# Eleven buffers for the normalised rows of attention, and the MLP's first rows prepared inside the last expert tile

## The reference

```python
# attention: 8 heads of 64; heads 0-3 see the 32 positions before, heads 4-7 every 32nd position
scores = scale * np.matmul(q, k.transpose(0, 1, 3, 2))
scores = np.where(masks[None], scores, -1e9)
scores = scores - np.max(scores, axis=-1, keepdims=True)
attn = np.exp(scores)
attn = attn / (np.sum(attn, axis=-1, keepdims=True) + 1e-09)
x = np.matmul(attn, v)            # rearranged to (2304, 512)
# experts: rows with x @ w_skip > 0 go to one of 8 experts, the others pass through
h = np.maximum(x[mask] @ w1[e], 0.0)
out[mask] = x[mask] + gate_w[mask, None] * (h @ w2[e])
# MLP, 512 -> 2048 -> 512
h = out @ w_in
g = np.maximum(0.01 * h, h)
return g @ w_out
```

## Time and profile before

| | |
|---|---|
| timed runs, median (lowest to highest) | 775.16 us (774.77 to 778.14), 3 runs |
| the profiled execution: its time | 770.74 us |
| its span, first to last instruction | 768.8 us |
| TensorE, matmuls busy | 719.7 us (94%) |
| VectorE, ScalarE, GpSimd busy | 276.0, 231.6, 182.8 us |
| mean granted TensorE clock | 0.973 of full speed |

### The profile page before, as it was taken

One profiled execution on the slowest core, in us unless ns is written; L12 is line 12 of the kernel. 1 busy time (PEld: TensorE's weight loads), 2 busy tenths in 40 slices (PEclk: granted clock), 3 DMA queues, 4 the chain that ended last, 5 costly groups with the idle time before them and its releaser, 6 DMA issues.

```text
span 768.8 us, 12332 instructions
## 1 busy us (share of the span) xinstructions
PE 719.7 (94%) x4674; PEld 670.2 (87%) x4674; DVE 276.0 (36%) x597; ACT 231.6 (30%) x505; POOL 182.8 (24%) x173
## 2 busy tenths in 40 slices
PE   4979999594989999998999999999999999999997
PEld 3969999583989999997999999999999999899986
DVE  5736667467431111113233223323222322232222
ACT  2645676251111111112222322222222232223222
POOL 5231110002267777764000300110030002001000
PEclk9988999796899999999999999999999999999999
DMA  8475755852777999961000200010020002001001
GB/s 177 111 176 123 179 144 156 245 183 67 239 227 259 318 311 319 310 225 58 3 1 1 83 0 1 29 55 1 0 74 8 0 7 75 0 0 42 1 1 41
DMA packets 68648, 81.68 MB, mean 106 GB/s; under 512 B 26137, under 2 KB 47417, under 8 KB 68602
## 3 DMA queue, kind: packets, MB, share of 16 engines
q1 hardware_dynamic: 60040, 58.60, 25.5%
q0 software_dynamic: 7504, 22.44, 9.0%
q10 hardware_dynamic: 1058, 0.02, 0.1%
HBM read 68.84 MB, written 12.21 MB: 105 GB/s over the span
## 4 chain that ended last, share of the span: by engine, by line
PE 83%; DMA 6%; DVE 4%; SPq 2%; issue 2%; ACT 1%; POOL 0%; ACTq 0%; DVEq 0%; POOLq 0%
PE psum L1643 26%; PE psum L1661 26%; PE psum L1537 9%; PE psum L1553 8%; DMA x_rows<-xo 5%; PE psum L1414 3%; PE psum L1435 2%; PE psum L1386 2%; SPq L447 1%; PE psum L1476 1%; PE psum L1493 1%; PE psum L1424 1%; PE psum L1563 1%; PE psum L1625 1%; PE psum L1405 1%
## 5 line engine op out<-in xcount | busy, mean ns | idle before, releaser
L1353 DVE SCALAR_TENSOR_TENSOR g_act<-g_raw 128x384 f32<-128x384 f32 x96 | 53.5, 558 | 230.9 <-ACT g_raw L1004 230.9
L1643 PE MATMUL psum<-x2h,wih 128*128 128x384 f32 x384 | 130.6, 340 | 2.4 <-DVE x2l L1335 2.4
L1643 PE MATMUL psum<-x2h,wil 128*128 128x384 f32 x384 | 129.4, 337 | 0.0
L1643 PE MATMUL psum<-x2l,wih 128*128 128x384 f32 x384 | 128.9, 336 | 0.0
L1004 ACT ACTIVATE g_raw<-psum 128x384 f32<-128x384 f32 x96 | 47.2, 492 | 235.6 <-PE psum L1643 235.6
L1661 PE MATMUL psum<-woh,g_l 128*128 128x512 f32 x288 | 114.0, 396 | 0.0
L1661 PE MATMUL psum<-wol,g_h 128*128 128x512 f32 x288 | 113.8, 395 | 0.0
L1661 PE MATMUL psum<-woh,g_h 128*128 128x512 f32 x288 | 112.2, 389 | 0.6 <-DVE g_l L1357 0.6
L844 POOL DMA_INDIRECT out_dram<-o_sb,idxo x15 | 16.0, 1064 | 294.4 <-ACT o_sb L999 291.3
L1537 PE MATMUL psum<-xt,wring 128*128 128x160 f32 x512 | 82.6, 309 | 0.6 <-issue 0.6
L1553 PE MATMUL psum<-hp,wring 128*128 128x160 f32 x512 | 78.2, 301 | 0.0
(11 more groups left out here) (208 smaller groups left out, 875.8 us busy)
## 6 DMA issues: line engine op xcount, KB each, us to landing
wring<-in_moe_w_dram SPq DMA_DIRECT2D x64, 512.0 KB, 5.7
x_sb<-x_rows SPq DMA_DIRECT2D x4, 1024.0 KB, 7.3
stage<-in_moe_w_in_dram POOLq DMA_DIRECT2D x4, 1024.0 KB, 5.5
stage<-in_moe_w_out_dram POOLq DMA_DIRECT2D x4, 1024.0 KB, 8.2
q_st<-in_q_dram SPq DMA_DIRECT2D x7, 576.0 KB
k_st<-in_k_dram SPq DMA_DIRECT2D x7, 576.0 KB
vs<-in_v_dram SPq DMA_DIRECT2D x20, 128.0 KB, 7.9
x_rows<-xo SPq DMA_DIRECT2D x8, 288.0 KB, 7.0
```

The costliest lines, as they stand in the source:

```text
L1353: dve.scalar_tensor_tensor(out=g_act[:, f % 2, :], in0=g_raw[:, f % 2, :], scalar=LEAK, in1=g_raw[:, f % 2, :], op0=ALU.mult, op1=ALU.max) ...
L1643: last = pe.matmul(bank[f % 2][:, 0:MT * P], wt[:, c, f * P:(f + 1) * P], xp[:, T.par, c, :], start=(c == 0 and n == 0), stop=(c == KD - 1 ...
```

## The change

- `xo` has a slot for each of the 11 groups. `normalised` waits for the store of its own slot of the batch before, no longer for one of its own batch. The regions behind it in SBUF move up by five slots.
- On POOL, in tile 8, the gather of the MLP's first rows comes first, behind a wait for the split before it (s_stl), and ahead of tile 7's put.
- `tile(0, E - 1, ends=True)`: TensorE turns the three row blocks inside it, two behind share 5, one behind share 6, the third into bank 0 instead of bank 7 (`X2T_0`); ScalarE and VectorE split them there, ahead of the copies of y.
- y of tile 8 is turned in the MLP, behind share 0 of its first block (banks 2 and 3); `rows_of_eight` on VectorE is its x2_rows, behind g_l of step 1; POOL's put waits for it (s_r8).
- g_h moves to the second half of `stage`, so ScalarE waits once for the last split; the loads of last_tile and last_par from the plan move into the overflow part, which redoes gather, turn and split (this part, with semaphores s_t2, s_h2, s_l2r, is not entered here and is cut below).

```diff
-    xo = at(a, "xo", [P, NL, 4 * DH])
+    xo = at(a, "xo", [P, NG, 4 * DH])
...
+    m_ = [a2[0] + 2048 * 4]
+    g_h = at(m_, "g_h", [P, 2, MT * P], F32R)
     m_ = [a2[0] + 2 * 2048 * 4]
     o_sb = at(m_, "o_sb", [P, MT, D])
-    g_h = at(m_, "g_h", [P, 2, MT * P], F32R)
+    m_ = [a2[0] + 2 * 2048 * 4 + 2 * 2 * D * 4]
...
+        X2T_0 = [bank[i] for i in (2, 3, 0)]
...
-                src = xo[0:G["m"], g - NL, :]
+                src = xo[0:G["m"], g, :]
...
+                if i == 2 * NU - 1:
+                    pool.wait_ge(s_srt, 16)
+                    pool.wait_ge(s_stl, i)
+                    indices(0)
+                    gather_rows(s_gm)
                 if i == 0:
                     pool.wait_ge(s_xt, 2)
...
-                if i == 2 * NU - 1:
-                    pool.wait_ge(s_srt, 16)
-                    indices(0)
-                    gather_rows(s_gm)
                 stage_split(i)
...
             with pool.Else():
-                pool.sem_inc(s_rd, 1)
-                pool.wait_ge(s_x2r, 2 * E)
+                pool.wait_ge(s_r8, 2)
                 put_x(E - 1)
...
+                if ends:
+                    for j in range(MT):
+                        x2_hi(0, j, 0)
                 act.wait_ge(s_l2, T.n(FC, FC))
...
+                    if T.first and f == 0:
+                        act.wait_ge(s_stl, 2 * NU)
...
-                if o < NL:
-                    dve.wait_ge(s_xs[store_of(o + NL if o + NL < NG else o)], 16 * b + 16)
-                else:
-                    dve.wait_ge(s_xs[store_of(o - NL)], 16 * b + 32)
+                dve.wait_ge(s_xs[store_of(o)], 16 * b + 16)
...
+            def rows_of_eight():
+                dve.wait_ge(s_y8, 2)
+                dve.tensor_copy(gate2[:, :], gate_s[:, 2 * (E - 1):2 * E]).then_inc(s_g8, 1)
+                dve.wait_ge(s_g8, 1)
+                dve.wait_ge(s_yf, E)
+                for hf in range(2):
+                    dve.scalar_tensor_tensor(out=yr[:, hf, :], in0=bank[2 + hf][0:HALF, :],
+                                             scalar=gate2[:, hf:hf + 1],
+                                             in1=xg[:, (E - 1) % 2, hf, :], op0=ALU.mult,
+                                             op1=ALU.add).then_inc(s_r8, 1)
...
+                if ends:
+                    for j in range(MT):
+                        x2_lo(0, j, 0)
                 dve.wait_ge(s_l2, T.n(FC, FC))
...
-            x2_rows(last_tile, last_par, 5)
-            for j in range(MT):
-                x2_lo(0, j, 0)
...
+                    if f == 1 and T.first:
+                        rows_of_eight()
...
+                    if ends and f == FC - 1:
+                        pe.wait_ge(s_x2r, T.n(2, 0))
+                        x2_turn(0, 0)
+                        x2_turn(0, 1)
+                    if ends and f == FC:
+                        x2_turn(0, 2)
...
-            pe.wait_ge(s_yv, last_tile + 1)
-            y_turn(last_tile, 5)
-            pe.wait_ge(s_x2r, last_tile * 2)
-            pe.wait_ge(s_rd, 1)
-            for j in range(MT):
-                x2_turn(0, j)
...
-                    pe.wait_ge(s_x2r, tiles * 2)
...
+                    if T.first and f == 1:
+                        y_turn(E - 1, s_y8)
+                    if T.first and f == 7:
+                        pe.wait_ge(s_r8, 2)
```

More of the change, by code:

```diff
@@ L531, in _, with tile @@
             tiles = sp.value_load(plan[0:1, 31:32], min_val=E, max_val=TILES)
-            def tile(i0, d):
+            def tile(i0, d, ends=False):
                 nxt = i0 + (d + 1)
@@ L551, in _ @@
                     tile(i2 * 2, u + 1)
-            tile(0, E - 1)
+            tile(0, E - 1, ends=True)
             with sp.If(tiles > E):
@@ L967, in _ @@
                     tile(Tile(i2 * 2, u + 1))
-            tile(Tile(0, E - 1), False)
+            tile(Tile(0, E - 1), False, ends=True)
             with act.If(tiles > E):
@@ L1297, in x2_rows, with x2_lo, tile @@
                                              op1=ALU.add).then_inc(s_x2r, 1)
-            def tile(T, ahead=True):
+            def x2_lo(m, j, par, made=s_m3h, done=s_m3l):
+                dve.wait_ge(made, m * MT + j + 1)
+                dve.tensor_tensor(x2l[:, par, :, P * j:P * j + P],
+                                  x2_bank(m, j).rearrange("d (c t) -> d c t", c=KD),
+                                  x2h[:, par, :, P * j:P * j + P].bitcast(F32),
+                                  ALU.subtract).then_inc(done, 1)
+            def rows_of_eight():
[8 more added lines that the diff above has]
+                                             op1=ALU.add).then_inc(s_r8, 1)
+            def tile(T, ahead=True, ends=False):
                 first, par = T.first, T.par
@@ L1562, in y_turn, with x2_turn, tile @@
                     for c in range(KD):
-                        last = pe.transpose(bank[to + hf][0:HALF, c * P:(c + 1) * P],
+                        last = pe.transpose(bank[2 + hf][0:HALF, c * P:(c + 1) * P],
                                             yt[:, c, HALF * hf:HALF * hf + HALF], ident[:, :])
-                    last.then_inc(s_yt, 1)
-            def tile(T, ahead=True):
+                    last.then_inc(s_done, 1)
+            def x2_turn(m, j, landed=None, turned=s_m3):
+                pe.wait_ge((landed or s_gm)[j], m * 16 + 16)
+                for c in range(KD):
+                    last = pe.transpose(x2_bank(m, j)[:, c * P:(c + 1) * P],
+                                        x3[:, j, c * P:(c + 1) * P], ident[:, :])
+                last.then_inc(turned, 1)
+            def tile(T, ahead=True, ends=False):
                 first, par = T.first, T.par
@@ L1599, in _ @@
                     tile(Tile(i2 * 2, u + 1))
-            tile(Tile(0, E - 1), False)
+            tile(Tile(0, E - 1), False, ends=True)
             with pe.If(tiles > E):
+                pe.wait_ge(s_m3l, MT)
                 for hf in range(2):
```

57 lines of the change are left out of this document (32 added, 25 removed).

## The result

| | before | changed kernel |
|---|---|---|
| median, 20 runs each on one chip | 777.27 us | 769.83 us |
| ratio, 95% interval | | 0.9922 (0.9901 to 0.9943) |
| profiled execution: time, span | 770.74, 768.8 us | 769.87, 767.9 us |
| mean granted clock of that execution | 0.973 | 0.973 |

A ratio of 0.9922 is 6.1 us less (4.4 to 7.7); 6.4 us had been forecast, and a time of 768.8. One slow run of the changed kernel (778.85) is left out of the ratio, which stays close to that of the means; the two medians differ by 7.4 us. The two profiled executions differ by 0.9 us only, so the profile has two things to tell: where the gain is, and why this pair hides most of it.

A forecast was written before the change was run, and what follows sets the result against it. Bounds: xo store waits in attention with SP's load queue close behind, and TensorE's waits at the expert-to-MLP seam. Gains 3.8 + 2.6 = 6.4 us, taken off the 775.16 median, gave 768.8 us, own range 767.5 to 769.7.

The forecast's parts named there:

- SP wins 1.3 us: SP's load queue in attention: without two waits for xo, later loads are issued 1.3 us earlier, ends 0 and 1.76.
- Attention without its waits ends near 138 to 140: End of attention: TensorE finishes by 140 and idles from about 138 until batch 0's rows arrive.
- Batch 0's rows at 144.8: Start of routing: batch 0's rows land at 144.8 instead of 146.1, and routing starts there.
- Block 13 at 162.1, 3.8 us won: Routing's first row block needing batch 3 starts at 162.1 instead of 165.95, 3.8 us won out of 16.
- part 1: Attention's end: eleven slots for xo bring 3.8 us, ends 2.6 and 6 us.
- After block 13 routing goes on as before: Rest of routing: stays bound by TensorE as before, so the 3.8 us won at block 13 are kept.
- the clock falls again: Rival at block 13: TensorE's idling brings 1.2 GHz back and takes 5 us, 1.4 us won, 773.8; chance 0.14.
- The signs of being wrong: Last x_load much before 154 or after 156.5, routing's clock low beyond 10 us, or seam over 2 us.
- Gathers and put on POOL cost nothing: POOL in the last tile: earlier gathers hide in idle time, puts hardly move, the split behind starts 4.8 us earlier.
- Turns in the tile 1.34 us, then 1.20 us for the step: Last expert tile: twelve transposes cost 1.34 us; stepping over the not-taken overflow block delays the MLP 1.20 us.
- y in the MLP 0.81 us: MLP behind share 0: eight y transposes cost TensorE 0.81 us in full.
- The seam 2.6 us: Between last expert tile and MLP: 3.43 us earlier start less 0.81 is 2.6 us won, ends 1.4 and 3.2.

The follow-up runs named there:

- run 2: Changed kernel with six xo slots and the old waits for them, so the seam's part alone, against the kernel before: ratio 0.9960, 3.1 us.
- run 1: Kernel before with the eleven xo slots and nothing else, against the kernel before: ratio 0.9955, 3.5 us.
- run 3: Changed kernel without the overflow part (not entered here) and its branch on TensorE; ratio to the kernel before 0.9884.
- run 7: Changed kernel with turns of the identity on TensorE, 30 before block 0 and 12 before block 13; ratio to the kernel before 0.9945.
- run 8: The changed kernel measured once more, nothing altered; ratio to the kernel before 0.9891.
- run 11: Changed kernel with 30 and 12 turns of the identity before blocks 0 and 13, without TensorE's overflow part; ratio to the kernel before 0.9861.
- run 12: run 5 with 20 turns of the identity on TensorE before block 13; ratio to the kernel before 0.9827.
- Run 4: Changed kernel with x_load of batches 0, 1 and 2 issued on ScalarE's queue instead of SP's; ratio to the kernel before 0.9891.
- run 9: run 5 with SP's x_load of batches 0 and 1 moved into batch 2, and of batch 2 to group 4 of batch 3; ratio 0.9859.
- run 10: run 9 without the overflow part on TensorE (not entered here); ratio to the kernel before 0.9876.
- run 5: Changed kernel with the v loads of batch 3's last three groups issued by POOL instead of SP; ratio to the kernel before 0.9860.
- run 6: run 5 without the overflow part on TensorE (not entered here); ratio to the kernel before 0.9866.

## Why the prediction was right, point by point

- *SP wins 1.3 us.* 1.31 in the pair of profiles, by luck: the last x_load was issued at 156.85 and 156.29 with six slots (before, run 2) and at 153.6 to 157.1 with eleven (changed kernel, runs 1, 3, 7, 8 and 11, mean 155.2), so 1.4 us on average with up to 2 to either side from one execution to the next. That the DMA rings are full beside the two gaps of SP's queue, as the prediction has it, no row shows; the rows show issues of 0.8 to 0.9 us there and a DMA share of 0.90 (46 to 53) and 0.95 (80 to 88).
- *Attention without its waits ends near 138 to 140.* Its last values stood at 138.27 to 139.5, but not by TensorE's pace: the v loads of the last groups held it for 4.6 us. The text had SP's queue close behind VectorE for x_load and did not follow it to the v loads. It cost nothing, because x_load was later still.
- *Batch 0's rows at 144.8.* They came at 146.1 in this profile (143.8 in run 8), nothing gained there; it did not matter, as block 13 decides.
- *Block 13 at 162.1, 3.8 us won.* 161.95, 4.0 us; 160.0 to 163.6 over six profiles (those with eleven slots and SP's own order of loads). The step that 12 of 16 us do not arrive was right, and run 1 gives 3.5 us for all of part 1.
- *After block 13 routing goes on as before.* This step failed in three of the four profiles without the turns of the identity and with eleven slots on SP (changed kernel 11.79 us, run 1 10.23, run 3 10.24; run 8 8.66), for 8.57 before. It was the rival "the clock falls again", held at 0.14 and with 5 us; it takes 1.7 us on average of the four. Against that block 13 is 4.3 us early on average of the six, not 3.8, so 2.6 us are left; run 1's interval holds this as well as 3.8. The term of 3.8 us is thus right in size only: the prediction counted the idle time in front of block 13 as free, and it cost clock behind it.
- *The signs of being wrong.* One of them came true in the changed kernel: routing's granted clock is low beyond its first 10 us (routing starts at 146.14, and the clock is 0.53 and 0.50 from 163.5 to 170.4). A second, the last x_load after 156.5, came true in run 1 (157.08). The forecast time held all the same, by luck in so far as the 1.7 us lost behind block 13 are small beside the spread of the timed runs.
- *Gathers and put on POOL cost nothing.* The three gathers went out at 333.65 to 337.4, the split behind the puts began at 340.00 in a tile that stood 1.38 us later than before, so 4.8 us earlier, as forecast.
- *Turns in the tile 1.34 us, then 1.20 us for the step.* From the first of the 24 weight loads to the tile's last it grew from 21.57 to 22.90 us, 1.33; the step took 1.44, and 1.24 to 1.73 over the other profiles that have it. Run 3 shows that it was rightly put on the path: without it the start is 0.9 us earlier.
- *y in the MLP 0.81 us.* 0.87. yr ended at 362.63, the next block's gathers were out by 373.45 (forecast 371.4), and its turns had no wait.
- *The seam 2.6 us.* 3.20 - 0.87 = 2.33 by the trace, 3.1 (1.6 to 4.6) by run 2.
- *Where the profile and the runs differ.* The sum was made against an execution 4.4 us under its median, and only the cut was carried over. That was the right use of it: the first profile pair shows 0.9 us, the pair with run 8 7.9, the timed runs 6.1.

## What to carry to other kernels

When a wait goes, follow the queue that starts the next stage, each kind of transfer on it, before counting the wait as won: here 16 us of idle and slow time at TensorE were 4 us at the block that waits for the last load. Winning in front of such a load buys idle time, and the idle time can cost more than itself in clock; a few cheap matmuls in the gap (run 12) gave back 6.4 us of routing. A timed difference of a few us should be read from many runs and explained from more than one pair of profiles.

## What the runs showed of the hardware

**The clock behind a short idle time.** From block 13 to the last routing row, by the idle time of TensorE in front of block 13: 1.32 us of idle, 8.66 us; 1.45, 11.79; 1.76, 10.24; 2.11, 10.23; 2.23, 11.80; 2.85, 15.09; 3.49, 13.27; 3.90, 13.08. With turns of the identity in the gap (0.64, 1.82 and 0.80 us of idle left) 8.65, 8.66 and 8.66. Run 4 had no idle time there and took 8.60. So each of the seven idle times from 1.45 to 3.90 us without the turns was followed by some 3 to 15 us at 1.2 GHz, and the one of 1.32 was not; 1.32 and 1.45, both of the same kernel, lie so close that what decides between them stays open. Of the changed kernel's timed runs that count in the ratio, those with a mean clock of 0.972 to 0.977 took 765.9 to 771.8 us, those with 0.962 to 0.970 took 773.0 to 777.0; where in those executions the low clock lay, no profile tells.

**Stops of several engines at once.** The four stops of 0.8 to 1.2 us in the expert tiles stood in the first profile of the changed kernel and in runs 9 to 12, and in none of runs 1 to 8, nor in the profile of the kernel before. Run 8 is the changed kernel itself, so its code alone does not make them; runs 1 to 4 and 9 to 11 have the same chip number, 14, so the chip alone does not either. The runs of the kernel before that go with the profiles that have them had medians of 777.27, 776.36 and 776.01, the others 772.09 and 774.12. That the stops cost the kernel before some 4 us there too would fit this and is not shown, as no profile of it has them. POOL does not stop: its issue of the stage load takes 0.83 us (307.50 above), as in run 8 (301.67), and its next instruction follows at once. The cause stays open.

**VectorE's copy beside POOL.** In the second tile a copy of 80x2 numbers takes 4.07 us. VectorE and POOL in the changed kernel:

```profile
215.22 4.52 POOL L658 TENSOR_TENSOR wil<-stage,wih 128x2048 fp32r<-128x2048 f32 x1
215.69 4.07 DVE L1303 COPY gate<-gate_s 80x2 f32 x1 [2.11 <-PE psum L1594]
```

It ends within 0.03 us of POOL's subtraction, in every profile; the same copy beside an idle POOL, at 361.02 in the MLP, takes 0.17 us. Not every copy is held: that of xt out of PSUM at 327.95 ran its usual 0.49 us beside the subtraction of 327.94 to 332.46. VectorE's yr waits for the gate copy and the next gather for yr (POOL's first at 222.08), and TensorE idles 1 to 3 us for that gather in all kernels here.
